# Attention with complex decay, then two expert layers: the order of the decay chain across ScalarE, VectorE and GpSimd

## What is computed

```
mag = sqrt(a_re^2 + a_im^2);  scale = min(mag, 0.999) / (mag + 1e-6)
a = (a_re + i*a_im) * scale                    # a complex decay per position and channel
for t in range(S):
    state = a[t] * state + k[t] (outer) v[t]   # complex state, 48x48 per head
    y[t]  = q[t] . real(state)
```

## Time and profile before

| | us |
|---|---|
| median of 3 runs (1036.9 to 1039.54) | 1037.17 |
| the profiled execution's own time | 1046.87 |
| its span on the core | 1044.9 |

### The profile page before, as it was taken

How to read it: one execution, slowest core, us unless ns; L and a number is a source line. 1 busy time by engine, 2 the same in 40 slices (tenths; PEclk the granted TensorE clock), 3 DMA queues, 4 the chain that set the end, 5 groups by cost and what they waited for, 6 DMA issues and landing times.

```text
span 1044.9 us, 17329 instructions
## 1 busy us (share of the span) xinstructions
PE 954.9 (91%) x5836; PEld 841.1 (80%) x5837; DVE 423.3 (41%) x742; ACT 459.1 (44%) x773; POOL 515.1 (49%) x429
## 2 busy tenths in 40 slices
PE   2789888999873999999999999999999999999995
PEld 0577777777762899999889888999999999999995
DVE  6668888887773423232233332222212122122110
ACT  7778887877661222232222223333333333333322
POOL 4134555655554755865875973242243342422432
PEclk9788999999996899999999999999999999999998
DMA  4613354331024243433542532010010010000000
GB/s 157 171 53 98 109 198 123 92 108 47 31 84 169 94 136 131 159 99 105 157 163 83 177 121 47 16 38 16 16 39 16 8 45 17 31 1 1 31 1 31
DMA packets 47191, 84.04 MB, mean 80 GB/s; under 512 B 23813, under 2 KB 36377, under 8 KB 44569
## 3 DMA queue, kind: packets, MB, share of 16 engines
q1 hardware_dynamic: 40984, 48.59, 15.6%
q0 software_dynamic: 6144, 34.65, 9.4%
HBM read 65.80 MB, written 17.38 MB: 80 GB/s over the span
## 4 chain that ended last, share of the span: by engine, by line
PE 74%; ACT 8%; DVE 6%; issue 5%; POOL 4%; SPq 1%; DMA 1%; POOLq 0%; DVEq 0%; ACTq 0%
PE bank L2077 19%; PE bank L2090 19%; PE bank L2035 10%; PE bank L2057 10%; POOL wm L1820 3%; PE bank L2045 2%; PE bank L1095 2%; PE bank L1110 2%; PE bank L1082 2%; PE bank L1112 1%; PE bank L1165 1%; PE bank L1074 1%; PE bank L1152 1%; PE bank L1138 1%; POOL wm L1818 1%
## 5 line engine op out<-in xcount | busy, mean ns | idle before, releaser
L1846 POOL TENSOR_TENSOR act_r<-act_f,act_r 128x512 fp32r<-128x512 f32 x96 | 124.4, 1296 | 260.4 <-ACT act_r L1905 257.8
L2090 PE MATMUL bank<-w_out_r,act_r 128*128 128x384 f32 x1152 | 217.7, 337 | 0.3 <-POOL act_r L1846 0.3
L2077 PE MATMUL bank<-x,w_in_r 128*128 128x512 f32 x864 | 216.7, 395 | 0.0
L2090 PEld LDWEIGHTS bank<-w_out_r,act_r 128*128 128x128 f32 x1152 | 204.8, 188 | 8.9 <-POOL act_r L1846 0.6
L1966 DVE TENSOR_TENSOR act_f<-bank,small 128x512 f32<-128x512 f32 x96 | 66.4, 692 | 292.7 <-ACT small L1902 275.3
L2077 PEld LDWEIGHTS bank<-x,w_in_r 128*128 128x128 f32 x864 | 159.5, 188 | 29.5
L1902 ACT ACTIVATE small<-bank 128x512 f32<-128x512 f32 x96 | 57.4, 598 | 191.5 <-PE bank L2077 191.4
L2035 PE MATMUL bank<-wm,x_tr 128*128 (+1 forms) x522 | 129.3, 402 | 3.9 <-POOL wm L1820 1.7
L2057 PE MATMUL bank<-wm,h_tr 128*128 (+1 forms) x696 | 128.6, 339 | 0.8 <-DVE h_tr L1950 0.7
L2057 PEld LDWEIGHTS bank<-wm,h_tr 128*128 128x128 f32 x696 | 120.0, 188 | 1.3 <-issue 1.3
L2035 PEld LDWEIGHTS bank<-wm,x_tr 128*128 128x128 f32 x522 | 97.8, 192 | 24.9 <-issue 5.0
(11 more groups left out here) (193 smaller groups left out, 1428.3 us busy)
## 6 DMA issues: line engine op xcount, KB each, us to landing
stage<-moe_w POOLq DMA_DIRECT2D x12, 1536.0 KB, 7.1
qkv_in<-in_qkv SPq DMA_DIRECT2D x24, 576.0 KB, 5.6
a_in<-in_a SPq DMA_DIRECT2D x11, 768.0 KB
stage<-moe_w SPq DMA_DIRECT2D x4, 1536.0 KB
x_b<-x_sorted SPq DMA_DIRECT2D x30, 193.0 KB
y_sorted<-y_b SPq DMA_DIRECT2D x29, 192.0 KB
xg<-y_sorted SPq DMA_DIRECT2D x24, 192.0 KB, 2.4
stage<-w_out POOLq DMA_DIRECT2D x2, 1536.0 KB, 7.2
```

The lines of the kernel that those rows point to most:

```text
L1846: pool.tensor_tensor(a[:, 1, :], act_f[f % 2][:, :], a[:, 0, :].bitcast(F32), ALU.subtract).then_inc(s_gl, 1)
L2077: last = pe.matmul(h_bank[f % 2][:, :], w_in_r[:, wp, t * F2 + f * P:t * F2 + (f + 1) * P], window_part(w, xp)[:, t, :], start=(t == 0 and ...
L2090: last = pe.matmul(o_bank[j][:, 0:W], a[:, ap, j * P:(j + 1) * P], w_out_r[:, wp, f * W:(f + 1) * W], start=(f == 0 and n == 0), stop=(f = ...
```

## The change

The comment on the change: logarithm and exponential from one table set, falls of both chunks of a pair in one group, GpSimd's SBUF passes set beside VectorE's PSUM passes.

- ScalarE: the set with both logarithm and exponential is loaded ahead of `logs`, and `epsilon` runs from it at the start of the even iteration. Then comes a load of the set with exponential and tanh, the falls of both chunks of the unit, and `cosine_tanh`. In the odd iteration the sine's set is loaded first, then `angle`, `sine` and so on. There are no falls in odd iterations.
- The falls run one chunk further ahead: chunks n + 4 and n + 5 in an even iteration n (`fallen(n)`), with 4 buffers each in place of 3.
- VectorE: `cap`, `decay_log` (even) and `turns` (odd) move ahead of `scale(n + 1)`; `half_tangent` stands ahead of `phases`.
- TensorE: both `sum_logs` of a unit stand after `scores(n, 1)` in the even iteration and write the banks of the transposed k and q; `transposes(n, 0)` of an odd n waits for both rises.
- GpSimd: `sine_eps` waits until `scale` of the next chunk has run, `carry_in` until `scale` of the even chunk ahead has; in the odd iteration `decay` comes first, then both `carry_in`, and most of the routing's `tally` moves to there.
- SyncE: both `chunk_end` of the unit in the even iteration.

```diff
-    FALLS = 3
+    FALLS = 4
+    def fallen(n):
+
+        if n == 0:
+            return [2, 3, 4, 5]
+        return [n + 4, n + 5] if n % 2 == 0 and n + 4 < NCH else []
+
     def cum_of(m, part):
 
+        if part == 0 and m > 3:
+            return qt_bank if m % 2 else kt_bank
         return {(0, 1): kt_bank, (1, 0): sc_bank, (1, 1): qt_bank, (2, 0): u_bank}.get((m, part), cum_bank)
...
-            if n == 0:
-                chunk_end(2)
+            for m in fallen(n):
+                chunk_end(m)
             for m in summed(n):
-                chunk_end(m)
                 chunk_phase(m)
...
+            if u >= 3:
+                pool.wait_ge(s_qe, 2 * u - 4)
             pool.tensor_tensor(im, im, eps_mag[pair(u)][:, ucols(u)], ALU.mult).then_inc(s_sine_eps, 1)
...
             pool.wait_ge(s_turn, unit_of(m) + 1)
+            pool.wait_ge(s_qe, m - 1 - m % 2)
...
         for n in range(NCH + 1):
-            for m in summed(n):
-                carry_in(m)
+            if n % 2 == 1:
+                decay(n - 1)
+                for m in summed(n) + summed(n + 1):
+                    carry_in(m)
+            if n % B == 1 and B < n < NCH - 4:
+                pool.wait_ge(s_k, 9)
+                tally(n // B - 1)
             u = chain_exp(n)
             if u is not None:
                 cosine_log(u)
                 sine_eps(u)
-            decay(n - 1)
+            if n % 2 == 0:
+                decay(n - 1)
...
-                tally(g)
+                if n == NCH - 4:
+                    tally(g)
...
     def scan_scalar(act):
-        act.preload_act_table_set("natural_log")
+        act.preload_act_table_set("natural_log_exp_and_others")
...
         logs(1)
+        epsilon(0)
+        epsilon(1)
         squares(2)
         logs(2)
+        epsilon(2)
+        act.preload_act_table_set("exp_and_others")
         for u in range(2):
-            epsilon(u)
             cosine_tanh(u)
-        epsilon(2)
...
-        act.preload_act_table_set("natural_log")
+        act.preload_act_table_set("natural_log_exp_and_others")
         logs(3)
...
                 out_copy(n - 1)
+                if u is not None:
+                    epsilon(u)
                 query(n, 1)
                 rows(n - 1)
-                if n == 0:
-                    falls(2)
-                for m in summed(n):
+                if u is not None:
+                    act.preload_act_table_set("exp_and_others")
+                for m in fallen(n):
                     falls(m)
                 if u is not None:
-                    epsilon(u)
                     cosine_tanh(u)
...
             else:
-                for m in summed(n):
-                    falls(m)
                 u = chain_trig(n)
                 if u is not None:
                     act.preload_act_table_set("trig_and_small")
+                if chain_angle(n) is not None:
+                    angle(chain_angle(n))
+                if u is not None:
                     sine(u)
                 query(n, 1)
+                if u is not None:
+                    phase_size(u)
                 rows(n - 1)
                 if u is not None:
-                    phase_size(u)
                     cosine(u)
-                u = chain_angle(n)
-                if u is not None:
-                    angle(u)
...
                     squares(u)
-                    act.preload_act_table_set("natural_log")
+                    act.preload_act_table_set("natural_log_exp_and_others")
...
+            if chain_exp(n) is not None:
+                cap(chain_exp(n))
+                decay_log(chain_exp(n))
+            if chain_angle(n) is not None:
+                turns(chain_angle(n))
             scale(n + 1)
             if n % 2 == 0:
                 rotate(n + 1)
                 mask(n, 1)
                 u = chain_exp(n)
                 if u is not None:
-                    cap(u)
+                    half_tangent(u)
                 for m in summed(n):
                     phases(m)
-                if u is not None:
-                    decay_log(u)
-                    half_tangent(u)
...
             else:
                 rotate(n + 1)
-                u = chain_angle(n)
-                if u is not None:
-                    turns(u)
                 mask(n, 1)
...
         def sum_logs(m):
             pe.wait_ge(s_nl, unit_of(m) + 1)
-            if m >= 3:
-                pe.wait_ge(s_ph, m)
+            if m == 3:
+                pe.wait_ge(s_ph, 3)
+            if m > 3:
+                pe.wait_ge(s_kt[1], m - 3 - m % 2)
+                pe.wait_ge(s_qt, 2 * (m - 3 - m % 2))
...
             need(pe, s_carried, m - B + 1)
-            if m >= 2:
-                pe.wait_ge(s_rise, m + 1 if m >= 3 else 1)
+            if m in (2, 3):
+                pe.wait_ge(s_rise, 1 if m == 2 else 4)
+            if m > 3:
+                pe.wait_ge(s_ph, m)
...
             need(pe, s_kt[1 - h], n + h)
+            if h == 0 and n % 2 == 1 and n + 3 < NCH:
+                pe.wait_ge(s_rise, n + 5)
...
             scores(n, 0)
-            if n % 2 == 0:
-                for m in summed(n):
-                    sum_logs(m)
+            if n == 0:
+                sum_logs(3)
             transposes(n, 1)
...
             scores(n, 1)
+            for m in fallen(n):
+                if m > 3:
+                    sum_logs(m)
             outputs(n, 0)
...
             outputs(n, 1)
-            if n % 2 == 0:
-                for m in summed(n + 1):
-                    sum_logs(m)
```

## The result

The changed kernel takes 1025.77 us (median of 4 runs, 1016.53 to 1026.99); the kernel before takes 1037.94 us in the same comparison (1036.9 to 1039.54). The ratio is 0.9849, with a 95% interval from 0.9817 to 0.9881, so it is faster by about 1.5%. The forecast was 1019 with a range from 1010 to 1030: the time lies in it, but 7 us above the point. The profiled execution takes 1026.31 us, where the one before took 1046.87. The profile thus shows 20.6 us of gain and the medians show 12, because the profiled execution of before was slower than its own median and that of after was not.

The account below looks back on a forecast made before the run. Attention stage bound by waits among three nearly full engines, TensorE's floor 20.8 us a pair; 11.4 + 2.8 + 2 - 0.3 gives 16, plus 2 of dips, 18 us: median 1037.17 to 1019, range 1010 to 1030.

Parts of the forecast that it names:

- Plain pairs: Attention-stage iteration pairs 0, 2, 4, 8, 12, 16, without rank products: forecast 21.4 us against 23.3, 1.9 less each.
- The term of 0.35 us for a stall at sum_logs: Even iteration: VectorE reaches decay_log late behind numerator and add_update, so TensorE stalls 0.35 us; bounds 0 and 1.3.
- The term of 0.2 for the transposes: Odd iteration: gaps of 0.88, 0.60 and 0.96 us become one of about 0.2 ahead of the transposes; bounds 0 and 1.2.
- rival A: Attention stage: gaps and slow-clock dips go wholly, 24 us and up to 27 gained, 1010 to 1014 us; chance 0.17.
- pair with ranks: Four attention-stage pairs holding the routing's two rank products: forecast 23.1 us, 0.7 less each.
- 0.35 + 0.75 = 1.1 us: Stall at sum_logs where ranks run: 0.35 us from VectorE arriving late, 0.75 from positions ahead of cap awaiting the ranks.
- At sum_turns it had 0.7: Where ranks run, GpSimd's scatter ahead of decay and carry_in makes sum_turns wait 0.7 us; scatter bounds 0 and 2.
- the dips' 8 us: Attention-stage pairs where the granted clock falls to half hold about 8 us; a quarter, 2 us, was counted as gone.
- B: Cap meets GpSimd's cosine_log and costs 1.53 us, not 0.55, in every pair: 9.8 us given back, about 1028; chance 0.16.
- C: The wait for the falls only moves to the transposes and takes the odd iteration's gain: 1036 to 1039 us; chance 0.08.
- D: The falls' wait moves to the transposes and grows, late epsilon delaying decay_log, sum_logs and falls: about 1050 us; chance 0.07.
- The name of the change is no gain by itself: ScalarE: the combined table set still leaves three loads of 1.28 us a pair; only the last falls lose theirs.

Follow-up runs that it names:

- the fastest kernel: The changed kernel with positions moved behind cap and decay_log and GpSimd's two scatters moved behind the carries, in pairs with ranks: 1010.76 us, ratio 0.9711 to the kernel before.

## Why the prediction was right, and where it was not

**The mechanism held.** The odd iteration's wait for the falls is gone: ScalarE's timeline of after has the sine's load right behind k's copy, with no idle time where the earlier trace rows had 1.59 us, and angle ahead of sine as the prediction had it.

```profile
136.28 0.58 ACT L702 ACTIVATE k_t<-bank 96x512 f32<-96x512 f32 x1
136.88 1.28 ACT L792 ACT_TABLE_LOAD   x1
138.18 0.85 ACT L655 ACTIVATE main<-main 128x768 f32<-128x768 f32 x1
```

Three loads a pair stayed, as said, and all behind the attention stage took the same time within 1.3 of 707 us.

**Plain pairs: the cost was too high.** Forecast 21.4, measured 20.70 in three of five (20.41 and 21.74 in iterations 2 and 4). The term of 0.35 us for a stall at sum_logs was 0 in these three, and 0.43 and 0.42 us in iterations 2 and 4; there cap takes 0.99 us, and 0.55 in the three. The term of 0.2 for the transposes was there in all five, with 0.29 to 0.34. The other part of the miss is TensorE's own work: 20.28 us busy in the pair shown above, where the prediction took all of 20.8 that was left beside the three gaps. What the prediction gave no term is VectorE's relief. Its instances in after, 60 to 250 us (minimum, median and maximum ns):

```profile
L826 DVE CUSTOM_DVE_ANT_0 log_sq<-main,log_sq,least_run x8: 1007/1009/1742, 76.2 to 238.2; 128x768 f32<-128x768 f32 x8
L833 DVE TENSOR_SCALAR flip<-a_in x8: 546/546/803, 75.7 to 237.7; 128x768 f32<-128x768 f32 x8
L847 DVE TENSOR_SCALAR neglog<-log_sq x9: 546/559/993, 61.0 to 244.9; 128x768 f32<-128x768 f32 x9
```

The same three passes took on average 1.58, 1.03 and 0.91 us before, in the same stretch. The prediction had this only in rival A, as "up to 27 with VectorE's passes shorter"; it gave the waits on GpSimd no term. Taken out of the fastest kernel they cost 27 to 28 us, which says how much that kernel's order leans on them, but not by how much the sum was off.

**The stalls of the pair with ranks.** At sum_logs the prediction had 0.35 + 0.75 = 1.1 us, and all four pairs show 1.20. At sum_turns it had 0.7, and the gaps are 1.13, 1.00, 1.00 and 0.66. All waits of TensorE of this kind together, from 60 to 250 us of after (us in total, times, longest):

```profile
PE bank L1095 <- DVE neglog L854: 5.7, 6, 1.2
PE bank L1105 <- issue: 3.1, 3, 1.1
PE bank L1135 <- DVE qr L910: 2.8, 8, 0.4
```

A pair with ranks and no slow clock takes 23.25 us, where 23.1 was forecast. The last two rows are the first scores of iterations 16 and 18, and the prediction set the first of them, read from the chain, against a start read from the timeline; by the timeline alone that pair took 23.69 before, not 23.86, so its gain is 0.44 us and not 0.7.

**The step that failed is the slow clock.** "Of the dips' 8 us I take a quarter as gone: the gaps they follow mostly go." In the plain pairs they went wholly, and in iteration 0's in part. But the change opens gaps of 1.0 to 1.2 us in the pairs with ranks, and the prediction, which had just sized them at 1.1 and 0.7, gave them no slow clock. They brought 7.7 us of it. With the gaps filled by unread products the kernel is 6.6 us faster, and with the gaps mostly or wholly taken away 9.6 and 13.4. Without this one effect the time would have been 1017.5, close to the 1019 forecast; the further 7 us, in the fastest kernel, are the gaps themselves. What rival A wanted, 1010 to 1014, is what that kernel reaches.

**The rivals.** B, cap beside `cosine_log`, is there in part: in after cap is 0.99 us at worst and 0.65 on average, not 1.53 in every pair. In the fastest kernel, where VectorE comes earlier, it is 1.07 on average and leaves gaps of 0.17 to 0.35 us, and 0.71 once, so this rival was waiting behind the gaps that it replaces. C and D, the wait that only moves to the transposes, are refuted for the changed kernel, where the transposes wait for rotate alone. With decay_log some 4 us late no transposes waited for a rise either, though the slow clock behind sum_logs gives the falls more time there, and the kernel was nevertheless slower than before. The slower side was real, but its place is sum_logs itself, which stands on TensorE ahead of the outputs, and not the rises behind it.

**"The name of the change is no gain by itself"** was wrong. The number of loads stayed, as said, but the place of one is worth 9 to 13 us. Not tried was the logarithm's own set with epsilon behind q's copy, so the 9 to 13 us belong to the order tested and not to every order without the combined set.

**Turns and the end.** Turns ahead of the rotations was taken as worth the gap of 0.96 us; undone it costs 16 us: this gap, 9.5 us, and 4.3 more at sum_logs from GpSimd passes that have moved beside VectorE's, less 4.7 at the transposes; slow clock behind some of the gaps is in the rest. The end of the stage gave 2.8 us where 2 was forecast. The start of iteration 0's scores did not move by the forecast 0.3 us (34.10 before, 34.05 after).

The sum was 18 us against the profiled execution's 20.6 and the medians' 12.2. The first is near because two misses cancel, which is luck and not a right sum. The plain pairs and iteration 0's gave 23.6 us, where 11.4 and 2 for the dips had been forecast, and the end and all behind it gave 4.1 where it had been 2; the pairs with ranks lost 7.1 where 2.8 were to be won. The gap between 20.6 and 12.2 is a reason not to transfer a gain read from one profiled execution to medians without a bound of its own.

## What to carry to other kernels

A wait added to an engine with time to spare can be worth more than the whole change brought (27 to 28 us here, against 12), when it keeps that engine's SBUF reads away from VectorE instructions that have two inputs in SBUF: look for one shape with two durations in the trace, and order the work so that only the instructions with an input in PSUM meet it. When a change empties some stretches of gaps and opens a gap of about 1 us in others, price the granted clock at the new gap too: here it cost some 1.5 us behind a gap of 1.0 to 1.2, as much again as the gap and more. A table load costs by what stands behind it in the queue, so a combined set pays even where the number of loads stays.

## What was not expected of the hardware

- A VectorE product that writes PSUM and reads two SBUF tensors takes 2.17 us beside a GpSimd pass and 0.56 without one. A conversion of 128x4 values takes 1.65 us beside one and 0.17 without. The time stands inside the instruction's duration; no view of waits shows it.
- Gaps of TensorE of 1.20 us were followed by a stretch at 1.2 GHz in place of 2.4 GHz (granted clock 0.66 over 5 us) in three of four pairs, at the same places in two executions. In the fourth, at 246.46 us, the same gap brought none, and a gap of 1.14 us at sum_turns brought none either once the one ahead of sum_logs in the same pair was short. A gap of 1.55 us ahead of transposes in iteration 21 has slow clock behind it in the changed kernel (0.73 from 280 to 285 us) and none in the kernel with the fills. What makes the difference stays open.
- Filling such a gap with products that nothing reads makes the kernel 6.6 us faster; on the kernel before, where the filled gap was 0.96 us, it brought nothing that can be measured.
